# Moving one product of the normalisation to GpSimd, earlier weight pieces, and part of the first constant products in array halves

## The chip, the cores and the metric

One core of one Trainium2 chip runs the whole program: five engines (TensorE, VectorE, ScalarE, GpSimd, and SyncE that issues transfers), each with its own instruction stream, and semaphores between them. The metric is the time of one execution on the device in microseconds; the comparison uses the median of several runs.

## What is computed

The reference is a chain of three parts over 2304 tokens of width 512, all in float32.

```python
# 1: linear attention, 4 batches, 8 heads, 576 tokens, head size 64, 128 features
proj = x @ w_phi ; proj -= max(abs(proj)) ; phi = [exp(proj), exp(-proj)]
out = phi(q) @ (phi(k).T @ v) / (phi(q) @ sum(phi(k)) + 1e-6)
# 2: one of 8 experts per token (argmax of x @ w_gate)
x = gate * sigmoid(...) * (relu(x @ w1[e]) @ w2[e])          # 512 -> 1024 -> 512
# 3: RMS norm and a gated FFN
xn = x / sqrt(mean(x * x) + 1e-6) * rms_g                    # rms_g: one factor per feature
y  = (silu(xn @ w_gate) * (xn @ w_val)) @ w_out              # 512 -> 1536 -> 512
```

With these inputs only three experts are chosen by any token.

## The kernel before

Every large product is made of three products of split operands: a value is stored as a high part (rounded, type fp32r) and a low part (value minus high part), and high*high, high*low and low*high are added in PSUM. ScalarE writes high parts, VectorE writes low parts. So each tile that TensorE reads has passed ScalarE and then VectorE.

**Start.** `keep_warm(n)` (line 774) issues n products of a constant tile `warm` with 512 columns each; their results are never read. Twelve stand before the first slot of attention, eight between slots 0 and 1, eight between slots 1 and 2 (lines 779 to 786). The first slot waits for loads, for the split of `w_phi` and for the first tile of k.

**Attention** runs in slots, one per 128 tokens of k or q; rows are scattered to DRAM by expert in the end.

**Experts.** Tokens of an expert are taken in tiles of 288 (G). One tile is one *step*; there are eight steps g = 0 to 7 in this run, step 0 ahead of the routing table, then three *turns* (one per expert) of one, four and two steps. In a step TensorE goes through eight chunks m of 128 hidden rows: `hidden(m)` (12 products, lines 833 to 835), then `outputs(m-2)` (12 products, lines 846 to 848). `hidden(m)` needs VectorE's `relu_low(m-2)`, `outputs(m)` needs `relu_low(m)`. The next tile is transposed in four parts: `next_transpose` 0 and 1 after `hidden(7)`, 2 and 3 after `outputs(5)`; part 2 goes to the PSUM bank of part 0 and so waits until `take_rows` has read part 0 on ScalarE and VectorE. `once` (a turn's start) waits until all eight weight pieces of the turn are split.

**Weight pieces.** The next expert's weights are split in eight pieces during the first step of a turn (`split_step`, with `split` given): ScalarE `split_high` (line 975), VectorE `split_low` (line 1317), one piece at each of chunks 0 to 5 and two behind the last `take_rows`. Two such steps are in the experts' stage: g = 1 and g = 2. GpSimd issues the loads: `raw_in(2, ...)` (line 613) for the second matrix of the turn after the next once all eight pieces are split.

**Normalisation of tile n = g-1** runs inside step g in the same streams:
- ScalarE `copy_out` (1051): PSUM to `x2g` [128, 4, 288], at the start of the step.
- GpSimd `add_squares` (581, 584, 587): squares and two sums; TensorE `sum_squares` (854) after `hidden(4)`; VectorE `mean` (1386) at chunk 3; ScalarE `root` (1056) at chunk 3.
- VectorE `normal` at chunk 4: `reciprocal` (1391), then four products x2g * g * inverse root in place (1397).
- ScalarE `normal_high` at chunk 5: one copy of 1152 elements to `xoH` (1062). VectorE `normal_low` at chunk 5: `xoL` = x2g - xoH (1405).
- SyncE `rows_out` (465, 468, 472): stores xoH, then xoL, then the token numbers (a DRAM to DRAM transfer of 4 byte elements).

**Entry to the FFN.** The FFN's weights are twelve blocks of [128, 3, 512]. Blocks 0 and 1 pass through the buffer `stage[0]`, block 2 through `stage[1]`, which lies where expert weights were. SyncE's order after the loop is written by hand:

```python
e.wait_ge(s["pe_s1"], last * FC + 1)
block_in(0)                       # stage[0]
e.wait_ge(s["xst"], total * 32)
group_in(0)                       # first 384 tokens
e.wait_ge(s["pl_b"], 2)           # block 0 split, stage[0] free
block_in(1)
rows_out(prior)                   # tile 6
e.wait_ge(s["pe_s2"], total * FC + 2)
e.dma_start(stage[1], ffn_w[2])
for i in range(3, NF): block_in(i)    # each waits for bk_lo >= i - 2
```

GpSimd splits block 0 (lines 644, 646) behind its last step; ScalarE and VectorE split the others (1137, 1549) between the parts of group 0. `ffn_up(i)` (926 to 928, 24 products) waits for block i, `ffn_down(i-1)` (940 to 942) follows it. Six groups of 384 tokens, twelve blocks each, fill the rest of the time.

Of the kernel before, what the change touches and what calls it, by code (L numbers as in the profile page):

```python
# [25 lines left out]
P = 128  # L26
# [15 lines left out]
G = 288  # L42
# [16 lines left out]
def build_program(nc, q, k, v, w_phi, wg, wog, w1, w2, ffn_w, rms_g, out):  # L59
# [8 lines left out]
    with ctx:  # L68
# [88 lines left out]
        def sb(name, shape, dt=F32):  # L157
# [80 lines left out]
            "normalised, split, stored; token numbers stored, read": "dve_xn act_xh dve_xl xst idst id_in id_c",  # L238
# [84 lines left out]
        split_slots_dve = [(B - 1, sl) for sl in (1, 2, 3, 6, 8, 9)] + [(B, 0), (B, 1)]  # L323

# [50 lines left out]
        def _(e):  # L375
# [82 lines left out]
            def rows_out(n):  # L458
# [7 lines left out]
                e.wait_ge(s["dve_xl"], n + 2)  # L466
# [58 lines left out]
        def _(e):  # L525
# [93 lines left out]
            def step(par, g):  # L619
                add_squares(g - 1)  # L620
                gate_rows(g + 1)

            def split_step(pair, par, g):
# [3 lines left out]
                gate_rows(g + 1)  # L627
                with e.If(has_turn(pair * 2 + (par + 2))):
# [6 lines left out]
            with e.If(early > 0):  # L635
                e.sem_inc(s["pl_sq"], 1)
                e.sem_inc(s["pl_s0"], 1)
                e.sem_inc(s["pl_ss"], 1)
            with e.If(early < 1):
                gate_rows(0)  # L640
# [7 lines left out]
            add_squares(total_steps(e) - 1)  # L648
# [8 lines left out]
        def _(e):  # L657
# [120 lines left out]

            e.wait_ge(s["c_warm"], 1)
            keep_warm(12, (YM, YM + 1, YM + 2, YM + 3))  # L780
# [3 lines left out]
            keep_warm(8)  # L784
# [181 lines left out]
        def _(e):  # L966
# [101 lines left out]
            def step(par, g, split=None):  # L1068
                table(ACT.Sqrt)
                copy_out(g - 1)  # L1070
                for m in range(FC):
                    if m == FC - 1:
                        take_rows(g + 1, XT_BANK, (0, 1))
                    relu(g, m)
                    if split is not None and m < FC - 2:
                        split(m)
                    if m == 3:
                        root(g - 1)
                    if m == 5:
                        normal_high(g - 1)  # L1080
# [51 lines left out]
            def block_high(i):  # L1132
                if i == NF - 1:
                    e.wait_ge(s["dve_xl"], total + 1)
# [50 lines left out]
        def _(e):  # L1185
# [202 lines left out]
            def normal(n):  # L1388
# [3 lines left out]
                e.wait_ge(s["pl_sq"], n + 2)  # L1392
                settle(e, "carry_dve")
                e.wait_ge(s["dve_R"], n + 2)
                settle(e, "carry_dve")
# [3 lines left out]
                last.then_inc(s["dve_xn"], 1)  # L1399

            def normal_low(n):
# [6 lines left out]
            e.sem_inc(s["dve_r"], 2)  # L1408
            over_batches(e, slot, NJ)
# [6 lines left out]
            with e.If(early > 0):  # L1416
                take_rows(0, XT_FIRST)
                for name in ("dve_ms", "dve_R", "dve_xn", "dve_xl"):
# [90 lines left out]
            def step(par, g, split=None):  # L1509
                for m in range(FC):  # L1510
                    if m == FC - 1:
                        take_rows(g + 1, XT_BANK, (0, 1))
                    relu_low(g, m)
                    if split is not None and m < FC - 2:
                        split(m)
                    if m == 3:
                        mean(g - 1)
                    if m == 4:
                        normal(g - 1)
                    if m == 5:  # L1520
                        normal_low(g - 1)
# [99 lines left out]
```

## Time and profile before

| what | value |
|---|---|
| median of 3 runs | 951.33 us (948.44, 951.33, 953.78) |
| the profiled execution's own time | 948.03 us |
| span of its instructions | 946.4 us |
| TensorE busy | 927.0 us, 98% |
| VectorE, ScalarE, GpSimd busy | 440.6, 303.6, 118.5 us |
| stages by TensorE's lines | attention to 259 us, experts 259 to 486, FFN 487 to 940 |

The span counts from the first to the last instruction; 1.6 us of the execution lie around it. Busy times of the other engines say little here, since each of them works in short bursts that TensorE may or may not wait for. What is read are TensorE's waits, and for each of them what the other engines and the transfer queue did just before.

### The profile page before, as it was taken

The numbers are of one execution on the slowest core, as the hardware profiler recorded it, in microseconds if no ns is written. First come the engines' busy times: TensorE is split into PE (matmuls) and PEld (weight loads), VectorE is DVE, ScalarE is ACT, GpSimd is POOL, SyncE is SP. The second block draws the span as 40 slices with busy tenths as digits, with TensorE's granted clock in tenths as the row PEclk, the third lists the DMA queues.
The fourth block names the chain that finished last, engine by engine and source line by source line (L and its number), as shares of the span: only waits on it lengthen the run. The fifth ranks groups of instructions, "written<-read, shape, count | busy, mean of one in ns | idle before, by whom it ended". The sixth has DMA issues, their size and how long they took to land.

```text
span 946.4 us, 16281 instructions
## 1 busy us (share of the span) xinstructions
PE 927.0 (98%) x6240; PEld 888.4 (94%) x6241; DVE 440.6 (47%) x869; ACT 303.6 (32%) x491; POOL 118.5 (13%) x135
## 2 busy tenths in 40 slices
PE   8999999999999899999999999999999999999996
PEld 7999999999999899999999899999999999999995
DVE  5667767678565764433356642222222222222221
ACT  4444444465315553222344422112112112112111
POOL 1000210201333311222420001001001001001001
PEclk9999999999999999999999999999999999999999
DMA  9620821500154843333753360011002002000000
GB/s 266 183 59 1 299 80 54 146 1 34 46 182 137 190 84 72 70 39 61 175 150 134 133 185 34 1 34 67 1 1 100 0 0 100 0 0 34 1 1 33
DMA packets 52960, 75.35 MB, mean 80 GB/s; under 512 B 26512, under 2 KB 42512, under 8 KB 51248
## 3 DMA queue, kind: packets, MB, share of 16 engines
q1 hardware_dynamic: 46816, 56.07, 23.3%
q0 software_dynamic: 3488, 17.85, 5.2%
q10 hardware_dynamic: 2608, 0.79, 0.4%
q8 instruction: 31, 0.51, 0.2%
q14 instruction: 17, 0.14, 0.0%
HBM read 51.06 MB, written 23.64 MB: 79 GB/s over the span
## 4 chain that ended last, share of the span: by engine, by line
PE 91%; DVE 3%; DMA 2%; ACT 2%; issue 2%; POOL 0%; POOLq 0%; SPq 0%; DVEq 0%; ACTq 0%
PE ps L926 10%; PE ps L928 10%; PE ps L927 10%; PE ps L696 8%; PE ps L713 7%; PE ps L941 5%; PE ps L942 5%; PE ps L940 5%; PE ps L833 3%; PE ps L834 3%; PE ps L846 3%; PE ps L835 3%; PE ps L848 3%; PE ps L847 3%; PE ps L670 3%; PE ps L672 2%
## 5 line engine op out<-in xcount | busy, mean ns | idle before, releaser
L926 PE MATMUL ps<-xnH,blkH 128*128 128x384 f32 x576 | 193.8, 337 | 1.4 <-issue 1.0
L928 PE MATMUL ps<-xnH,blkL 128*128 128x384 f32 x576 | 193.6, 336 | 0.0
L927 PE MATMUL ps<-xnL,blkH 128*128 128x384 f32 x576 | 193.4, 336 | 0.0
L1556 DVE TENSOR_TENSOR sg<-sg,ps 128x384 f32<-128x384 f32 x72 | 39.9, 554 | 247.5 <-ACT sg L1142 247.5
L1142 ACT ACTIVATE sg<-ps 128x384 f32<-128x384 f32 x72 | 35.4, 491 | 254.2 <-PE ps L928 254.2
L926 PEld LDWEIGHTS ps<-xnH,blkH 128*128 128x128 f32 x576 | 108.3, 188 | 5.6 <-issue 2.7
L927 PEld LDWEIGHTS ps<-xnL,blkH 128*128 128x128 f32 x576 | 108.3, 188 | 2.7
L928 PEld LDWEIGHTS ps<-xnH,blkL 128*128 128x128 f32 x576 | 108.3, 188 | 0.0
L940 PE MATMUL ps<-blkH,hH 128*128 128x512 f32 x216 | 84.6, 392 | 0.9 <-DVE hL L1560 0.9
L941 PE MATMUL ps<-blkL,hH 128*128 128x512 f32 x216 | 84.9, 393 | 0.0
L942 PE MATMUL ps<-blkH,hL 128*128 128x512 f32 x216 | 84.9, 393 | 0.0
L833 PE MATMUL ps<-xmH,w1H 128*128 128x288 f32 x256 | 77.3, 302 | 5.9 <-DVE hmL L1379 3.3
L846 PE MATMUL ps<-hmH,w2H 128*128 128x288 f32 x256 | 78.7, 307 | 0.0
L834 PE MATMUL ps<-xmL,w1H 128*128 128x288 f32 x256 | 76.8, 300 | 0.0
L835 PE MATMUL ps<-xmH,w1L 128*128 128x288 f32 x256 | 76.6, 299 | 0.0
L848 PE MATMUL ps<-hmH,w2L 128*128 128x288 f32 x256 | 75.7, 296 | 0.0
L847 PE MATMUL ps<-hmL,w2H 128*128 128x288 f32 x256 | 75.7, 296 | 0.0
L1192 DVE TENSOR_REDUCE mx<-ps 128x4 f32<-128x512 f32 (+1 forms) x80 | 54.8, 685 | 42.6 <-PE ps L672 42.3
L713 PE MATMUL ps<-kvs,ex 128*128 128x65 f32 (+1 forms) x640 | 71.8, 266 | 0.5 <-DVE x L1233 0.5
L652 POOL DMA_INDIRECT out_dram<-ysb,idI x18 | 17.4, 969 | 430.7 <-ACT ysb L1157 427.4
L713 PEld LDWEIGHTS ps<-kvs,ex 128*128 128x128 f32 (+1 forms) x640 | 69.2, 184 | 1.3 <-issue 1.2
L1379 DVE SCALAR_TENSOR_TENSOR hmL<-ps,hmH 128x288 fp32r<-128x288 f32 x64 | 29.2, 456 | 84.7 <-ACT hmH L1046 84.2
(197 smaller groups left out, 1658.8 us busy)
## 6 DMA issues: line engine op xcount, KB each, us to landing
stage<-in_ffn_w SPq DMA_DIRECT2D x12, 768.0 KB, 4.6
xin<-xs_dram SPq DMA_DIRECT2D x9, 578.2 KB, 10.1
xs_dram<-zrow SPq DMA_DIRECT2D x8, 578.2 KB, 8.1
qT<-in_q SPq DMA_DIRECT2D x4, 1152.0 KB, 6.5
xnH_dram<-xoH SPq DMA_DIRECT2D x8, 576.0 KB, 3.4
xnL_dram<-xoL SPq DMA_DIRECT2D x8, 576.0 KB, 5.3
xnH<-xnH_dram SPq DMA_DIRECT2D x6, 768.0 KB, 5.2
xnL<-xnL_dram SPq DMA_DIRECT2D x6, 768.0 KB, 6.3
```

Source lines behind the costliest of these rows:

```text
L713: last = e.matmul(NUM[0:n, h // 4, h % 4, :], ex[:, at[1] % 2, sign, h, 0:n], kvs[:, 2 * h + sign, :], start=(sign == 0), stop=(sign == 1))
L833: e.matmul(o, w1H[par][:, c, cols], xmH[:, c, :], start=(c == 0), stop=False)
L834: e.matmul(o, w1H[par][:, c, cols], xmL[:, c, :], start=False, stop=False)
L835: last = e.matmul(o, w1L[par][:, c, cols], xmH[:, c, :], start=False, stop=(c == KC - 1))
L846: e.matmul(o, w2H[par][:, m, cols], hmH[:, m % 2, :], start=(m == 0), stop=False)
L847: e.matmul(o, w2H[par][:, m, cols], hmL[:, m % 2, :], start=False, stop=False)
L926: e.matmul(o, hi, xnH[par][:, c, :], start=(c == 0), stop=False)
L927: e.matmul(o, hi, xnL[par][:, c, :], start=False, stop=False)
L928: last = e.matmul(o, lo, xnH[par][:, c, :], start=False, stop=(c == KC - 1))
L940: e.matmul(o, hH[:, i % 2, tok], blkH[i][:, 2, :], start=(i == 0), stop=False)
L941: e.matmul(o, hH[:, i % 2, tok], blkL[i][:, 2, :], start=False, stop=False)
L942: last = e.matmul(o, hL[:, i % 2, tok], blkH[i][:, 2, :], start=False, stop=(i == NF - 1))
```

## The change

- The four products of `normal` become one product on GpSimd (`normalise`), x2g * inverse root, in place, after `gate_rows` in GpSimd's step. VectorE keeps the reciprocal (`inverse`), now at chunk 5.
- The factor g moves into the last split: `normal_high` is four ScalarE instructions with a scale, `normal_low` four VectorE instructions (x2g * g) - xoH; both stand at the end of the step, behind `take_rows(2, 3)`. So `copy_out` of the next step waits for `normal_low` (`dve_xl`).
- The eight pieces stand at chunks 1 to 6 (`PIECES_AT`); none is left behind the last `take_rows`. `root` moves to chunk 4.
- Start: `keep_warm(12)` becomes `keep_warm(8)` and `keep_warm_tiles(3)`; the first `keep_warm(8)` between slots becomes `keep_warm(3)` and `keep_warm_tiles(3)`.
- In the FFN's group 0 VectorE does `inverse` where it did `normal`; GpSimd does `normalise` of the last tile behind its `add_squares`.

```diff
+        PIECES_AT = {1: (0,), 2: (1, 2), 3: (3,), 4: (4, 5), 5: (6,), 6: (7,)}
@@ SyncE, rows_out
-                e.wait_ge(s["dve_xl"], n + 2)
+                e.wait_ge(s["dve_xl"], n + 3)
@@ GpSimd
+            def normalise(n):
+                e.wait_ge(s["dve_R"], n + 2)
+                settle(e, "carry_pool")
+                e.tensor_tensor(x2g[:, :, :], x2g[:, :, :], rinv[:, :].unsqueeze(1).to_broadcast([P, KC, G]), ALU.mult)\
+                    .then_inc(s["pl_xn"], 1)
             def step(par, g):
                 add_squares(g - 1)
                 gate_rows(g + 1)
+                normalise(g - 1)
             def split_step(pair, par, g):
                 add_squares(g - 1)
                 with e.If(has_turn(pair * 2 + (par + 2))):
                     raw_in(1, pair * 2 + (par + 2), pair * (2 * PIECES) + ((par + 1) * PIECES + KC))
                 gate_rows(g + 1)
+                normalise(g - 1)
                 with e.If(has_turn(pair * 2 + (par + 2))):
                     raw_in(2, pair * 2 + (par + 2), pair * (2 * PIECES) + (par + 2) * PIECES)
...
-            add_squares(total_steps(e) - 1)
+            total = total_steps(e)
+            add_squares(total - 1)
+            normalise(total - 1)
@@ TensorE
+            def keep_warm_tiles(n):
+                plain = warm[:, :].bitcast(F32)
+                for _ in range(n):
+                    for at in (0, D):
+                        e.matmul(ps[at:at + D, XL, 0:P], plain[:, 0:D], plain[:, 0:P], start=True, stop=True)
+                for _ in range(n):
+                    for at in (0, D):
+                        e.matmul(ps[:, XL - at // D, 0:2 * P], warm[at:at + D, 0:P], warm[at:at + D, 0:2 * P],
+                                 start=True, stop=True)
-            keep_warm(12, (YM, YM + 1, YM + 2, YM + 3))
+            keep_warm(8, (YM + 3, XL))
+            keep_warm_tiles(3)
...
             slot(0, 0)
-            keep_warm(8)
+            keep_warm(3)
+            keep_warm_tiles(3)
             slot(0, 1)
@@ ScalarE
             def copy_out(n):
                 e.wait_ge(s["pe_s2"], n * FC + (FC + 2))
+                e.wait_ge(s["dve_xl"], n + 2)
...
-                e.wait_ge(s["dve_xn"], n + 2)
+                e.wait_ge(s["pl_xn"], n + 2)
                 e.wait_ge(s["xst"], n * 32 + 64)
-                e.activation(xoH[:, :, :], x2g[:, :, :], ACT.Copy).then_inc(s["act_xh"], 1)
+                for c in range(KC):
+                    last = e.activation(xoH[:, c, :], x2g[:, c, :], ACT.Copy, scale=gcol[:, c:c + 1])
+                last.then_inc(s["act_xh"], 1)
...
                 for m in range(FC):
+                    relu(g, m)
+                    if m == 4:
+                        root(g - 1)
+                    if split is not None:
+                        for n in PIECES_AT.get(m, ()):
+                            split(n)
+                    if m == FC - 2:
                         take_rows(g + 1, XT_BANK, (0, 1))
...
                 take_rows(g + 1, XT_BANK, (2, 3))
-                if split is not None:
-                    split(FC - 2)
-                    split(FC - 1)
+                normal_high(g - 1)
@@ VectorE
-                for c in range(KC):
-                    last = e.scalar_tensor_tensor(out=x2g[:, c, :], in0=x2g[:, c, :], scalar=gcol[:, c:c + 1],
-                                                  in1=rinv[:, :], op0=ALU.mult, op1=ALU.mult)
...
-                e.tensor_tensor(xoL[:, :, :], x2g[:, :, :], xoH[:, :, :].bitcast(F32), ALU.subtract)\
-                    .then_inc(s["dve_xl"], 1)
+                for c in range(KC):
+                    last = e.scalar_tensor_tensor(out=xoL[:, c, :], in0=x2g[:, c, :], scalar=gcol[:, c:c + 1],
+                                                  in1=xoH[:, c, :].bitcast(F32), op0=ALU.mult, op1=ALU.subtract)
+                last.then_inc(s["dve_xl"], 1)
...
                 for m in range(FC):
                     relu_low(g, m)
+                    if m == 5:
+                        inverse(g - 1)
+                    if split is not None:
+                        for n in PIECES_AT.get(m, ()):
+                            split(n)
                     if m == 3:
                         mean(g - 1)
+                    if m == FC - 2:
+                        take_rows(g + 1, XT_BANK, (0, 1))
                 take_rows(g + 1, XT_BANK, (2, 3))
+                normal_low(g - 1)
```

## Rows read from the trace of the kernel before

**Rows 1.** Waits of TensorE, whole span: who waits for whom, us in total, times, longest
```profile
PE ps L833 <- DVE hmL L1379: 3.3, 2, 2.0
...
PE ps L833 <- DVE w2L L1317: 1.2, 1, 1.2
...
PE ps L926 <- DVE blkL L1549: 0.3, 1, 0.3
```

**Rows 2.** Timeline of GpSimd, last expert step: start us, us, instruction, [idle before]
```profile
460.26 2.11 POOL L581 TENSOR_TENSOR sq<-x2g 128x1152 f32<-128x1152 f32 x1 [20.08 <-ACT x2g L1051]
462.55 1.43 POOL L584 TENSOR_TENSOR sq<-sq 128x576 f32<-128x576 f32 x1 [0.18 <-POOL sq L581]
...
469.54 1.47 POOL L644 CAST blkH<-stage 128x1536 fp32r<-128x1536 f32 x1
471.10 3.50 POOL L646 TENSOR_TENSOR blkL<-stage,blkH 128x1536 fp32r<-128x1536 f32 x1
```

**Rows 3.** Timeline of VectorE, last expert step
```profile
473.17 1.95 DVE L1391 RECIPROCAL rinv<-rinv 128x288 f32<-128x288 f32 x1
475.27 1.81 DVE L1397 SCALAR_TENSOR_TENSOR x2g<-x2g,gcol,rinv 128x288 f32<-128x288 f32 x4 [0.16 <-DVE rinv L1391]
476.99 0.45 DVE L1379 SCALAR_TENSOR_TENSOR hmL<-ps,hmH 128x288 fp32r<-128x288 f32 x1
```

**Rows 4.** Timeline of ScalarE, last expert step: relu of chunk 5
```profile
475.56 0.41 ACT L1046 ACTIVATE hmH<-ps 128x288 fp32r<-128x288 f32 x1 [2.79 <-PE ps L848]
```

**Rows 5.** Timeline of TensorE: first product of the FFN, first of block 2
```profile
487.15 0.41 PE L926 MATMUL ps<-xnH,blkH 128*128 128x384 f32 x1 [1.02 <-issue]
...
497.70 0.41 PE L926 MATMUL ps<-xnH,blkH 128*128 128x384 f32 x1
```

**Rows 6.** Timeline of SyncE's transfers, entry to the FFN: start us, us of issue
```profile
478.77 0.62 SPq L465 DMA_DIRECT2D xnH_dram<-xoH  x1
...
481.03 0.63 SPq L472 DMA_DIRECT2D ids_dram<-xs_dram  x1
486.23 0.34 SPq L507 DMA_DIRECT2D stage<-in_ffn_w  x1
```

**Rows 7.** Block 1, token numbers, block 2: KB, us from issue to landing
```profile
stage<-in_ffn_w SPq DMA_DIRECT2D x1, 768.0 KB, 4.3
...
ids_dram<-xs_dram SPq DMA_DIRECT2D x1, 1.1 KB, 9.1
...
stage<-in_ffn_w SPq DMA_DIRECT2D x1, 768.0 KB, 8.0
```

**Rows 8.** Timelines of ScalarE and VectorE: block 2's high part, block 1's low part
```profile
494.27 1.49 ACT L1137 ACTIVATE blkH<-stage 128x1536 fp32r<-128x1536 f32 x1 [0.46 <-DMA stage<-in_ffn_w]
...
488.12 1.76 DVE L1549 TENSOR_TENSOR blkL<-stage,blkH 128x1536 fp32r<-128x1536 f32 x1 [3.99 <-ACT blkH L1137]
```

**Rows 9.** Timelines of GpSimd and VectorE, step g = 1
```profile
303.94 2.03 POOL L574 TENSOR_SCALAR xin<-xin 96x512 f32<-96x512 f32 x3
...
304.41 2.64 DVE L1317 TENSOR_TENSOR w2L<-w2raw,w2H 128x1024 fp32r<-128x1024 f32 x1 [0.49 <-ACT w2H L975]
...
311.17 1.21 DVE L1317 TENSOR_TENSOR w2L<-w2raw,w2H 128x1024 fp32r<-128x1024 f32 x1
```

**Rows 10.** Timeline of TensorE: g = 1: transposes 0 and 1, transposes 2 and 3; start of the last turn
```profile
313.01 0.66 PE L798 MATMUL ps<-ident,xin 96*128 96x96 f32 x6
...
315.13 0.58 PE L798 MATMUL ps<-ident,xin 96*128 96x96 f32 x5
...
431.48 0.40 PE L833 MATMUL ps<-xmH,w1H 128*128 128x288 f32 x1 [0.47 <-issue]
```

**Rows 11.** Timeline of TensorE, start: constant products; then the second slot's second half
```profile
9.48 2.01 PE L777 MATMUL ps<-warm 128*128 128x512 f32 x8
...
12.39 0.38 PE L670 MATMUL ps<-wbdH,tH 128*128 128x256 f32 x1 [0.19 <-DVE pm L1199]
```

**Rows 12.** A window in attention: us, busy times PE, PEld, DVE, ACT, POOL (instructions), clock, DMA
```profile
187.60:191.00 3.40, 3.40 (x19) 3.40 (x17) 1.38 (x2) 1.18 (x2) 0.00 (x0) 0.50 0.02 5
```

More of the change, by code:

```diff
@@ L237, in build_program @@
                 "act_x2 pl_sq pl_s0 pl_ss pe_SS dve_ms act_rt dve_R",
-            "normalised, split, stored; token numbers stored, read": "dve_xn act_xh dve_xl xst idst id_in id_c",
+            "normalised, split, stored; token numbers stored, read": "pl_xn act_xh dve_xl xst idst id_in id_c",
             "FFN weights: loaded (one per staging buffer), split (the first block's on its own)":
@@ L638, in _ @@
                 e.sem_inc(s["pl_ss"], 1)
+                e.sem_inc(s["pl_xn"], 1)
             with e.If(early < 1):
@@ L1071, in step @@
                 for m in range(FC):
-                    if m == FC - 1:
-                        take_rows(g + 1, XT_BANK, (0, 1))
[L1074 to L1080, printed above, removed]
+                    relu(g, m)
[5 more added lines that the diff above has]
+                    if m == FC - 2:
+                        take_rows(g + 1, XT_BANK, (0, 1))
                 take_rows(g + 1, XT_BANK, (2, 3))
-                if split is not None:
-                    split(FC - 2)
-                    split(FC - 1)
+                normal_high(g - 1)
             def split_step(pair, par, g):
@@ L1133, in block_high @@
                 if i == NF - 1:
-                    e.wait_ge(s["dve_xl"], total + 1)
+                    e.wait_ge(s["dve_xl"], total + 2)
                     settle(e, "carry_act")
@@ L1386, in mean, with inverse @@
                 e.tensor_scalar(rinv[:, :], ps[:, RB, 0:G], 1.0 / DM, 1e-6, ALU.mult, ALU.add).then_inc(s["dve_ms"], 1)
-            def normal(n):
+            def inverse(n):
                 e.wait_ge(s["act_rt"], n + 2)
                 e.reciprocal(rinv[:, :], rinv[:, :]).then_inc(s["dve_R"], 1)
[L1392 to L1395, printed above, removed]
-                for c in range(KC):
-                    last = e.scalar_tensor_tensor(out=x2g[:, c, :], in0=x2g[:, c, :], scalar=gcol[:, c:c + 1],
-                                                  in1=rinv[:, :], op0=ALU.mult, op1=ALU.mult)
-                last.then_inc(s["dve_xn"], 1)
             def normal_low(n):
@@ L1417, in _ @@
                 take_rows(0, XT_FIRST)
-                for name in ("dve_ms", "dve_R", "dve_xn", "dve_xl"):
+                for name in ("dve_ms", "dve_R", "dve_xl"):
                     e.sem_inc(s[name], 1)
@@ L1510, in step @@
                 for m in range(FC):
-                    if m == FC - 1:
-                        take_rows(g + 1, XT_BANK, (0, 1))
                     relu_low(g, m)
-                    if split is not None and m < FC - 2:
-                        split(m)
+                    if m == 5:
[3 more added lines that the diff above has]
+                            split(n)
                     if m == 3:
                         mean(g - 1)
[L1518 to L1521, printed above, removed]
+                    if m == FC - 2:
+                        take_rows(g + 1, XT_BANK, (0, 1))
                 take_rows(g + 1, XT_BANK, (2, 3))
-                if split is not None:
-                    split(FC - 2)
-                    split(FC - 1)
+                normal_low(g - 1)
             def split_step(pair, par, g):
@@ L1571, in group @@
                         if i == 3:
-                            normal(total - 1)
+                            inverse(total - 1)
                         if i == 5:
```

1 line of the change is left out of this document (added).

## The prediction, made before the changed kernel was run

> **What bounds the kernel now.** I read four views, in this order. The page's busy times first: TensorE has 927.0 of 946.4 us, so only what delays TensorE counts, and little can be won. The waits of TensorE second [rows 1]: in the experts' stage it waits twice, 3.3 us in all (the longer 2.0, so the other 1.3), for VectorE's low part of the hidden rows, in the two steps that also split weights, and once, 1.2 us, for the last weight piece; in the FFN 0.3 us for a block. That is 4.8 us, the most that the change's aim can give. Third, the timelines at the entry to the FFN [rows 2 to 8], since the change puts new work on GpSimd there and SyncE's hand-written order waits for GpSimd. Fourth, the step with weight pieces [rows 9, 10] and the start [rows 11].
>
> **Entry to the FFN, the largest term.** The FFN's block 0 is split by GpSimd behind its last step. Before, its work there is done early: the high part at 469.54, the low part from 471.10 to 474.60 [rows 2]. With the change `normalise` of tile 6 stands ahead of it, and that waits for the reciprocal of the last step.
> - When the reciprocal ends: ScalarE's relu of chunk 5 runs 475.56 to 475.97 [rows 4], VectorE's low part takes 0.45, so 476.4, then 1.95 [rows 3]: 478.4. It was at 475.1, since it stood at chunk 4.
> - What `normalise` costs on GpSimd: no row shows it. The subtraction with two inputs took 3.50 for 1536 elements, the sum of two halves 1.43 for 576 [rows 2]; a line through both gives 1.43 + 576/960 * 2.07 = 2.67 for 1152. Lower bound 2.11, the square of the same 1152 elements from one input [rows 2]; upper bound 3.6, twice VectorE's 1.81 for the same product [rows 3]. I take 2.67, between its two nearest rows of two inputs. It ends at 481.1.
> - Block 0 then: 1.47 + 3.50 and 0.1 between [rows 2], so 486.2 in place of 474.60, 11.6 later. TensorE begins the FFN at 487.15 after 1.02 us in which it waited for nothing that the profile shows [rows 5]: covered, with 0.9 to spare.
> - Block 1 is the first loss. Its load waits for block 0 to leave the buffer: issue 486.2, landing 4.3 later [rows 7] at 490.5, high part 1.49, low part 1.76 [rows 8], ready at 493.8 (before 489.9). TensorE wants it after block 0's 24 products: between the two rows of [rows 5] it did 48 products of 384 columns and 9 of 512, 23040 columns in 10.55 us, so 24 of 384 take 4.2 and block 1 is wanted at 491.3. Stall 2.5.
> - Block 2 is the second. SyncE issues it behind `rows_out(6)`, and that now stands behind the wait of block 1's load. xoH goes out some 1.2 later at 487.4 (an estimate: about half the 2.26 between the issues of xoH and the token numbers), the numbers 2.26 after it at 489.7 [rows 6]. Before, the numbers landed 9.1 after their issue, at 490.1, and block 2, in the queue behind them since 486.23, at 494.2, that is 4.1 behind them [rows 6, 7]; ScalarE waited for it [rows 8]. Now: numbers landed at 498.8, block 2 at 502.9, split at 506.2. Before it was split at 497.5 (494.27 + 1.49 + 1.76) and TensorE took it at 497.70 without a gap. So 506.3 in place of 497.70: **+8.6**, the 2.5 of block 1 within it.
> - Bounds: 2.5 if block 2 doesn't wait behind the numbers (issue 490.5, landing 494.8, split 498.1, which the 2.5 already covers); 9.5 with the 3.6 for `normalise`.
> The Trainium skill, "GPSIMD Engine Reference", section Engine selection, sends elementwise products of two inputs to VectorE and has GpSimd at about half its speed; by that the product is the 3.6 of the upper bound and the sum 0.9 more. This case's rows put the price lower, no run has shown it yet.
>
> **The two steps with weight pieces.** VectorE loses the four products (1.81) from the chunks where it is late, and `normal_low` goes to the step's end. It gains pieces 6 and 7 there, 1.21 each [rows 9], for which it was free behind the last `take_rows` before. Let R be the end of the low part of chunk 5, on which `hidden(7)` waits. In its stream follow reciprocal 1.95, piece 6 1.21, low part of chunk 6 0.45, piece 7 1.21, low part of the first rows, of one chunk's size, 0.45: R + 5.3. GpSimd's work beside it is not free: beside `gate_rows` a piece took 2.64 in place of 1.21 [rows 9], so 1.4 more, and `normalise` now runs exactly beside pieces 6 and 7: R + 6.7. TensorE needs that low part for transposes 2 and 3: `hidden(7)` first, 1.6 (twelve products; twelve with six transposes take 2.12), then 2.12 from the first transposes to the second [rows 10]: R + 3.7. So the wait moves: not at `hidden(7)` any more but at transpose 2, up to 3.0, less what R comes ahead of the moment when TensorE wants it, which adding up chunks 4 and 5 puts at 0.3 to 0.5. I take 2.5 in each of two steps, 5.0 in place of 3.3: +1.7. The turn's start gains: pieces are all split, what is left is the overhead that the last turn's start shows (0.47 idle of its own [rows 10]) in place of 1.2: -0.7. Sum **+1.0**. Bounds: -4.0 (no wait left but that overhead) and +3.0 (another 1.4 from `gate_rows`, which slides to chunk 4 as SyncE's `rows_out` now waits for `normal_low` ahead of `rows_next`, and 0.6 in step 2).
> GpSimd issues the load of the second matrix (`raw_in(2)`) earlier, as all pieces are split before the step's end, though behind `normalise`; step 2 gets it in time. The other steps: `normal_high` (four times 0.41, overlapped) and `normal_low` (four times 0.45) lie behind `take_rows` and run under `outputs(6)`, `outputs(7)` and the first products of the next step; `copy_out` then ends about when ScalarE can begin relu 0. Cost nothing; if that cover goes, up to 0.3 in each of five steps. SyncE sends for the rows of the next tile later, since it waits for `normal_low` first; they are still gated ahead of `normalise`, and so ahead of the transposes.
>
> **FFN, group 0.** VectorE is 1.81 shorter ahead of block 6, whose low part TensorE waited 0.3 for [rows 1]: **-0.3**, bounds -0.7 and 0.
>
> **Start.** The first set is over before k's first tile is split, and TensorE idles there; the longer list fills that idle time: 0, at most +1.0 at the low clock. Second set: eight products of 512 columns took 2.01 with the last one's way through the pipe, 1.7 of issue, 0.21 each [rows 11]. Now three (0.64), six float32 ones of 128 columns and six of 256. In series, at float32's four passes, that is 6 * 0.21 + 6 * 0.11 = 1.9, in all 2.6: 0.85 more. 0.39 of it vanishes in the gap before the second half [rows 11] (0.19 idle and the rest of a start): **+0.5**. Bounds -0.1 and +1.2 (0.3 for each change of form unseen in the trace).
> The Trainium skill, "TensorEngine Tiling (Array Packing)", section Key Properties, says that tiles of the array run load and product in parallel; by that the second set takes 1.6 and this term is -0.1. No product of the trace before uses two halves at once, so the rows can't weigh it; TensorE's records will.
>
> **Sum** against the profiled execution's own 948.03: 8.6 + 1.0 - 0.3 + 0.5 = +9.8, 957.8. That execution lies 3.3 below the median of the three runs, 951.33. Part of the spread is the clock: three stretches of 3.41 us in attention and at the experts' start ran at 0.50 of full clock, 1.2 GHz in place of 2.4 [rows 12], each 1 to 1.7 us lost, and which stretches fall so need not repeat. The forecast is for the median: **961.1**. A measurement of this kernel can tell about 0.5% (4.8 us) from no change: below 946.6 and above 956.1.
>
> **Rivals.**
> - A, the forecast: blocks 1 and 2 both late. 0.65, 957 to 965.
> - B: the token numbers do not hold back block 2. For: they are 1.1 KB, and another pattern of the queue could let block 2 pass. Against: block 2 landed 8.0 after issue, 3.7 more than block 1 [rows 7]. Then 2.5 + 1.0 - 0.3 + 0.5 = +3.7, 955.0. 0.14.
> - C, the other side, not slower: GpSimd's product doesn't slow VectorE and the low part of the first rows comes by R + 3.7. The place is transpose 2 of steps 1 and 2, the price -4.0 in place of +1.0, and it decides the sign once the FFN's entry costs less than 4.3, so with B: 2.5 - 4.0 - 0.3 + 0.0 = -1.8, 949.5; if block 1 is early too, 947. For: VectorE is relieved of 1.81 where it was late. Against: 5.3 is over 3.7 even with no collision. 0.09.
> - D: the half-array products don't hold the clock, and the first slots run at 1.2 GHz for one more stretch of 3.41 us: +1.7 on A, or +3 with the shifted stretches of attention. For: the clock fell where TensorE's products were short [rows 12]. 0.12, 963 to 965.
>
> **Numbers.** Predicted 961.0. Range 953 to 966: from B less a microsecond or two to D. Faster by over 0.5%: 0.05 (C's better end and luck with the clock); within: 0.18 (B and the rest of C); slower: 0.77 (A, D, little of B).
>
> **What would show it.** Right: GpSimd's new product near 2.7 us at about 19.6 into a step; block 1 issued at about 27.5 into the last step in place of 15.9; TensorE waiting for `blkL` twice, some 2.5 and 6; ScalarE waiting for the `stage` transfer; a wait on the first rows' low part ahead of line 798 in steps 1 and 2; no w2L wait. Wrong: one wait of 2.5 only (B), none (block 0 still early), or no wait at line 798.

## The result, and the profile after

| kernel | median us | lowest to highest | runs |
|---|---|---|---|
| before | 952.34 | 948.44 to 953.78 | 4 |
| changed | 963.85 | 963.17 to 964.23 | 4 |

The row of before has the three runs given above and one more. The ratio is 1.0127, 95% interval 1.0094 to 1.0159: slower, by 11.5 us at the medians. The forecast was 961.0 in a range of 953 to 966. The profiled execution took 964.23. The changed kernel was timed once more later, beside others (below, changed_again): 959.17, ratio 1.0098.

The page of the changed kernel: span, busy times, and the slices with the granted clock.

```profile
span 962.5 us, 16361 instructions
...
PE 936.6 (97%) x6267; PEld 897.4 (93%) x6268; DVE 433.4 (45%) x861; ACT 307.9 (32%) x515; POOL 140.5 (15%) x143
...
PEclk9999999999799999999998999999999999999999
```

TensorE is busy for 936.6 of 962.5 us: 9.6 us more busy and 6.5 us more idle than before. The products are the same but for the start, so nearly all of the 9.6 is time at the lower clock, and the waits of TensorE (to be read against [rows 1]) hold the rest.

```profile
PE ps L953 <- DVE blkL L1568: 7.1, 2, 4.6
PE ps L825 <- DVE xmL L1400: 4.4, 2, 2.5
...
PE ps L860 <- issue: 1.4, 2, 1.0
PE ps L953 <- POOL blkL L658: 1.0, 1, 1.0
```

The waits of `hidden` for the hidden rows' low part (3.3) and for the weight piece (1.2) are gone, and so is the 0.3 at block 6. Two waits for the blocks of the FFN (7.1) and two for the low part of the next tile's first rows (4.4) stand in their place. The entry to the FFN, in the timelines of GpSimd, SyncE and ScalarE (against [rows 2, 6, 8]), and block 1 and 2 on TensorE (against [rows 5]):

```profile
484.53 2.66 POOL L595 TENSOR_TENSOR x2g<-x2g,rinv 128x1152 f32<-128x1152 f32 x1 [2.14 <-DVE rinv L1418]
487.13 1.47 POOL L656 CAST blkH<-stage 128x1536 fp32r<-128x1536 f32 x1
488.68 3.51 POOL L658 TENSOR_TENSOR blkL<-stage,blkH 128x1536 fp32r<-128x1536 f32 x1
```
```profile
492.22 0.36 SPq L489 DMA_DIRECT2D stage<-in_ffn_w  x1
494.42 0.62 SPq L467 DMA_DIRECT2D xnH_dram<-xoH  x1
...
496.31 0.66 SPq L474 DMA_DIRECT2D ids_dram<-xs_dram  x1
497.18 1.17 SPq L509 DMA_DIRECT2D stage<-in_ffn_w  x1
```
```profile
496.55 1.49 ACT L1164 ACTIVATE blkH<-stage 128x1536 fp32r<-128x1536 f32 x1 [3.62 <-DMA stage<-in_ffn_w]
...
509.28 1.48 ACT L1164 ACTIVATE blkH<-stage 128x1536 fp32r<-128x1536 f32 x1 [7.85 <-DMA stage<-in_ffn_w]
```
```profile
493.18 0.41 PE L953 MATMUL ps<-xnH,blkH 128*128 128x384 f32 x1 [1.01 <-POOL blkL L658]
500.18 0.66 PE L953 MATMUL ps<-xnH,blkH 128*128 128x384 f32 x1 [2.58 <-DVE blkL L1568]
```

The product on GpSimd takes 2.66 and pushes the split of block 0 to 487.13 to 492.2. TensorE takes it at 493.18, after 1.01 of idle time where it had 1.02 before [rows 5], so that itself costs nothing. Block 1's load leaves at 492.22, when that buffer is free, and TensorE takes block 1 at 500.18, after 2.58 of waiting. The token numbers leave at 496.31, block 2's load right behind them at 497.18, and ScalarE has it at 509.28. From issue to landing (against [rows 7]):

```profile
ids_dram<-xs_dram SPq DMA_DIRECT2D x1, 1.1 KB, 10.5
stage<-in_ffn_w SPq DMA_DIRECT2D x1, 768.0 KB, 12.1
```

TensorE reaches block 2 at 512.70 after 4.55 of waiting. From the FFN's first product to block 2 it took 19.52 us; before, 10.55 [rows 5].

**Where the 16.1 us of span went**, by TensorE's marks (the start of the experts, of the FFN, of block 2, the last product): up to the experts +3.5 (262.98 against 259.46), experts +2.5 (230.20 against 227.69), entry to block 2 +9.0, the rest +1.1. The windows at half clock account for most of the parts outside the entry; the last two lie within it or reach out of it.

```profile
185.90:189.30 3.40, 3.40 (x19) 3.40 (x17) 1.38 (x2) 0.78 (x2) 0.00 (x0) 0.50 0.00 0
247.30:257.50 10.20, 10.20 (x62) 9.71 (x61) 2.42 (x5) 1.19 (x2) 3.09 (x4) 0.50 0.00 0
261.00:267.80 6.80, 6.80 (x36) 6.54 (x35) 4.62 (x21) 1.86 (x5) 0.81 (x2) 0.50 0.37 89
349.70:353.10 3.40, 3.40 (x18) 3.32 (x17) 1.51 (x4) 2.92 (x7) 0.00 (x0) 0.51 0.00 0
499.90:503.30 3.40, 3.12 (x10) 3.15 (x11) 1.68 (x3) 0.52 (x1) 3.22 (x2) 0.50 1.42 136
510.20:517.00 6.80, 4.30 (x14) 4.33 (x15) 4.77 (x5) 2.83 (x4) 0.00 (x0) 0.50 0.37 136
```

The column behind the five engines is the granted clock as a share of 2.4 GHz. So 34 us of the span ran at 1.2 GHz, in the profile before 10.2 ([rows 12] is one of its three stretches). Three of these stretches began while TensorE waited or just after (349.70, 499.90, 510.20); the others lie where the change touches nothing.

### The profile page after: what moved, and what is told of

Read it like the earlier page. It is cut to its first block, busy times and chain, and to the rows that moved or that the text cites. A ratio compares the mean times of both kernels' runs of the same rounds, so it can differ in the third digit from the quotient of the medians.

```text
span 962.5 us, 16361 instructions
## 1 busy us (share of the span) xinstructions
PE 936.6 (97%) x6267; PEld 897.4 (93%) x6268; DVE 433.4 (45%) x861; ACT 307.9 (32%) x515; POOL 140.5 (15%) x143
## 4 chain that ended last, share of the span: by engine, by line
PE 92%; issue 2%; DMA 2%; DVE 2%; ACT 1%; POOL 1%; SPq 0%; POOLq 0%; DVEq 0%; ACTq 0%
PE ps L953 10%; PE ps L955 10%; PE ps L954 10%; PE ps L710 7%; PE ps L727 7%; PE ps L968 5%; PE ps L969 5%; PE ps L967 5%; PE ps L860 3%; PE ps L862 3%; PE ps L861 3%; PE ps L873 3%; PE ps L875 3%; PE ps L874 3%; PE ps L684 3%
## 5 line engine op out<-in xcount | busy, mean ns | idle before, releaser
L953 PEld LDWEIGHTS ps<-xnH,blkH 128*128 128x128 f32 x576 | 109.4, 190 | 12.4 <-issue 9.5
L727 PE MATMUL ps<-kvs,ex 128*128 128x65 f32 (+1 forms) x640 | 74.3, 272 | 0.0
L727 PEld LDWEIGHTS ps<-kvs,ex 128*128 128x128 f32 (+1 forms) x640 | 71.5, 190 | 0.9 <-issue 0.8
```

The source lines that it names most:

```text
L727: last = e.matmul(NUM[0:n, h // 4, h % 4, :], ex[:, at[1] % 2, sign, h, 0:n], kvs[:, 2 * h + sign, :], start=(sign == 0), stop=(sign == 1))
L953: e.matmul(o, hi, xnH[par][:, c, :], start=(c == 0), stop=False)
```

## The experiments

All ratios are against the kernel before, timed beside each of them in four sessions (medians 948.59, 950.94, 950.45 and 953.89; 17 to 29 runs each). "At equal clock" is explained under changed_again: it takes the run-to-run clock out, its unit is us above the kernel before, and its 95% intervals reach 0.4 to 0.8 to either side (0.2 for new_start_alone). The last column is from one profile of each kernel. quarter_product leaves work out, so its result is not that of the others.

| kernel | median us, runs | ratio (95%) | at equal clock | TensorE's waits for blocks; for first rows or hidden rows |
|---|---|---|---|---|
| changed_again | 959.17, 12 | 1.0098 (1.0067 to 1.0128) | +6.7 | 6.2; 4.2 |
| late_block0 | 958.46, 6 | 1.0096 (1.0067 to 1.0124) | +6.6 | 6.4; 2.7 |
| block2_ahead | 953.74, 10 | 1.0051 (1.0021 to 1.008) | +3.1 | 2.6; 4.1 |
| block0_first | 962.26, 7 | 1.0103 (1.0062 to 1.0144) | +5.4 | 6.1; 4.3 |
| rows_first | 956.47, 10 | 1.0058 (1.0028 to 1.0089) | +3.8 | 6.4; 0.4 |
| quarter_product | 955.28, 4 | 1.0068 (1.0041 to 1.0095) | +2.5 | 6.1; 0.7 |
| pieces_alone | 951.38, 10 | 1.0012 (0.998 to 1.0044) | +2.6 | 0.3; 5.8 |
| old_start | 960.99, 4 | 1.0116 (1.0066 to 1.0167) | +6.3 | 5.4; 4.0 |
| new_start_alone | 948.77, 10 | 0.9993 (0.9963 to 1.0023) | +0.2 | 0.3; 2.7 |
| all_three | 949.72, 10 | 0.9991 (0.9955 to 1.0026) | +0.6 | 3.4; 0.3 |
| tile6_behind_3 | 947.97, 12 | 0.9971 (0.9942 to 0.9999) | 0.0 | 3.1; 0.6 |
| tile6_behind_5 | 948.94, 12 | 0.9952 (0.9925 to 0.998) | -3.3 | none; 0.3 |

### Entry to the FFN

**late_block0**: the kernel before, with nothing of the change but the lateness of block 0.

```diff
+            late = total_steps(e)
+            e.wait_ge(s["dve_xl"], late)
+            settle(e, "carry_pool")
             e.wait_ge(s["st_0"], 16)
             e.tensor_copy(blkH[0][:, :, :], stage[0][:, :, :]).then_inc(s["pl_b"], 1)
```

> Kernel before, with one edit: GpSimd waits for the low part of tile 6 before it splits the FFN's block 0, so the split starts near 479.9 and ends near 485 in place of 474.6, still ahead of the moment when TensorE wants it. If the queue behind block 0 is the cause (block 1's load behind the split, block 2's load behind the token numbers), TensorE waits about 1.5 to 2.5 us for block 1 and 3.5 to 5 for block 2, and the kernel takes 5 to 8 us more than the kernel before, with no part of the change in it. If the late product itself or something else of the change makes the loss, it stays within 1 us of the kernel before.

Measured: 1.0096, and 6.6 at equal clock beside the 6.7 of the changed kernel. Block 0's split begins at 481.94 in place of 469.54 [rows 2]. The waits and the load of block 2:

```profile
PE ps L929 <- DVE blkL L1552: 6.4, 3, 4.7
PE ps L836 <- DVE hmL L1382: 2.7, 2, 2.0
```
```profile
502.66 1.48 ACT L1140 ACTIVATE blkH<-stage 128x1536 fp32r<-128x1536 f32 x1 [6.50 <-DMA stage<-in_ffn_w]
```

TensorE waits 1.4 at block 1 and 4.7 at block 2, with the product still on VectorE. So it is the time at which block 0 leaves its buffer that costs, through the chain of transfers behind it, whatever makes it late.

**block2_ahead**: the changed kernel, with block 2's load issued ahead of the stores of tile 6.

```diff
             block_in(1)
-            rows_out(prior)
             e.wait_ge(s["pe_s2"], total * FC + 2)
             settle(e, "carry_sp")
             e.dma_start(stage[1][:, :, :], ffn_w[2]).then_inc(s["st_1"], 16)
+            rows_out(prior)
```

> Changed kernel, with block 2's load issued right behind block 1's, ahead of the stores of tile 6 and its token numbers. If block 2 is late only because it queues behind the token numbers, its load lands some 5 us after its issue near 492.6, ScalarE no longer waits for it, and TensorE keeps only block 1's wait of about 2.6: 4.5 us less than the changed kernel from the wait and 1 to 3 more from the low clock that follows it. If block 2 were late for another reason (ScalarE or VectorE busy, the transfer itself slow), at most 1 us is won.

Measured: the second wait is gone, the first stays.

```profile
PE ps L825 <- DVE xmL L1400: 4.1, 2, 2.5
PE ps L953 <- DVE blkL L1568: 2.6, 1, 2.6
```

The entry took 14.89 (488.63 to 503.52) in place of 19.52, and the time fell by 3.6 at equal clock. The stores of tile 6 hold back the load behind them; rival B, by which block 2 would pass, falls.

This run moves all three stores, xoH and xoL of 576 KB each with the 1.1 KB of token numbers, and no run moves the numbers alone. In the changed kernel xoL itself took 10.6 from issue to landing (505.9), so the runs do not tell the three apart. The trace before tells more. There xoL had landed at 484.8 (issued at 480.02, 4.8 to landing), 1.4 before block 2's load was issued, and only the numbers were on their way, to 490.1; the load still took 8.0 where block 1's took 4.3 [rows 6, 7]. From 487.9 to 492.1 the 16 DMA engines were busy 45% of the time and moved 53 GB/s, from 492.1 to 494.5 they moved 405. So the bulk of the stores is not the cause there. The numbers are the likely one, but that was not shown by leaving them out.

**block0_first**: the changed kernel, with block 0's split inside the last step, after `gate_rows` and ahead of `normalise`, under a condition on the step's number.

```diff
             def step(par, g):
                 add_squares(g - 1)
                 gate_rows(g + 1)
+                block_0(g)          # split of block 0, if g is the last step
                 normalise(g - 1)
```

> Changed kernel, with block 0's split ahead of the new product in the last step alone. If GpSimd's order is the root of the entry's loss, block 0 is split by about 487.5 (5 after the rows are gated at 482.4), block 1 goes out some 4.5 us before TensorE's last expert product, and TensorE waits 0 to 1 us for block 1; block 2 still queues behind the token numbers, whose issue now follows the product that has moved back by about 2.5 (xoH near 493), so its wait stays at 4 to 7. So 2 to 4 us are won over the changed kernel, not all 7 to 9. If the order is not the root, nothing is won.

Measured: the wait at block 1 is gone (500.65 after 496.40, 4.25 as before), the one at block 2 grew from 4.6 to 6.1, and the entry took 16.77. Block 1 in time alone brings 1.3 at equal clock, with 0.8 to either side, less than the 2 to 4 expected: what TensorE no longer waits at block 1 it waits at block 2, which hangs on the stores of tile 6, and these on `normalise`. The two blocks are one chain, as the forecast put it ("the 2.5 of block 1 within it").

### The two steps with weight pieces

The steps of the changed kernel, on VectorE, GpSimd and TensorE in step g = 1 (against [rows 9, 10]):

```profile
314.50 1.16 DVE L1344 TENSOR_TENSOR w2L<-w2raw,w2H 128x1024 fp32r<-128x1024 f32 x1
315.58 0.44 DVE L1406 SCALAR_TENSOR_TENSOR hmL<-ps,hmH 128x288 fp32r<-128x288 f32 x1
315.94 3.29 DVE L1344 TENSOR_TENSOR w2L<-w2raw,w2H 128x1024 fp32r<-128x1024 f32 x1
319.15 0.81 DVE L1400 TENSOR_TENSOR xmL<-ps,xmH 128x288 fp32r<-128x288 f32 x2
```
```profile
314.76 3.39 POOL L595 TENSOR_TENSOR x2g<-x2g,rinv 128x1152 f32<-128x1152 f32 x1 [4.62 <-DVE rinv L1418]
```
```profile
319.74 0.80 PE L825 MATMUL ps<-ident,xin 96*128 96x96 f32 x6 [2.53 <-DVE xmL L1400]
```

Piece 7 takes 3.29 beside the product on GpSimd, where piece 6 just ahead took 1.16, and the product 3.39 in place of 2.66. The first rows' low part stands behind piece 7, and TensorE's transposes 2 and 3 wait 2.53 for it.

The records show in which way. Piece 6 ran beside the product too, from its start at 314.76 to 315.66, and was no longer for it. Piece 7 begins at 315.94, in the middle of the product; the product ends at 318.15 and piece 7 at 319.23, 1.08 later, which is nearly its whole length. Step g = 2 shows the same, 347.86 and 348.94 (start and duration of each added up):

```profile
344.45 3.41 POOL L595 TENSOR_TENSOR x2g<-x2g,rinv 128x1152 f32<-128x1152 f32 x1 [1.93 <-DVE rinv L1418]
345.63 3.31 DVE L1344 TENSOR_TENSOR w2L<-w2raw,w2H 128x1024 fp32r<-128x1024 f32 x1
```

So does the piece beside `gate_rows` before, 305.97 and 307.05 [rows 9]. By these records the two take turns: what begins second gets on at about the time when the other ends, and its price is what was then left of the other. No run was made for this alone. The short low part between the pieces (315.58), which reads PSUM, kept its 0.44.

**rows_first**: the changed kernel, with `take_rows(0, 1)` ahead of piece 7, on ScalarE and VectorE alike.

```diff
+                    if m == FC - 2:
+                        take_rows(g + 1, XT_BANK, (0, 1))
                     if split is not None:
                         for n in PIECES_AT.get(m, ()):
                             split(n)
-                    if m == FC - 2:
-                        take_rows(g + 1, XT_BANK, (0, 1))
```

> Changed kernel, with the first two parts of the next rows taken ahead of piece 7. If the wait at the transposes (2.5 and 1.9 us) comes from VectorE's queue, it goes, perhaps 0.5 us comes back at the second last output chunk, and the time falls by 3 to 4.5 us against the changed kernel. If it comes from the rows' load or from GpSimd's gating, it stays.

Measured: both waits of 2.5 and 1.9 are gone, 0.35 at `outputs(6)` and 0.82 at the turn's start are left, and 2.8 us are saved at equal clock. The entry's waits stay at 6.4.

**quarter_product**: the changed kernel, with the product on one of the four chunks of `x2g` (`x2g[:, 0:1, :]`, 288 elements in place of 1152); the other three leave the normalisation without the inverse root.

> Changed kernel with GpSimd's product on one of four chunks of the tile; the other three chunks leave without the inverse root. The product falls from 2.66 to about 0.8 us. If it slows the weight pieces beside it, piece 7 (3.3 us on VectorE) falls to 1.2 to 1.9 and the wait at the transposes from 2.5 and 1.9 to about 0.5 to 1 each. Block 0 is split 1.9 earlier, so block 1's wait falls from 2.6 to about 0.8; block 2's follows by up to 1.9. In all 4 to 6 us less than the changed kernel. If GpSimd and VectorE don't disturb each other, the wait at the transposes changes by under 0.5.

Measured, in step g = 1:

```profile
308.16 1.56 POOL L595 TENSOR_TENSOR x2g<-x2g,rinv 128x288 f32<-128x288 f32 x1 [4.62 <-DVE rinv L1418]
```
```profile
309.34 1.46 DVE L1344 TENSOR_TENSOR w2L<-w2raw,w2H 128x1024 fp32r<-128x1024 f32 x1
```

With 1.6 us of product in place of 3.4, piece 7 took 1.46 (it ended at 310.80, again 1.08 behind the product) and TensorE waited 0.7 once in place of 4.4: the length of the product beside the pieces makes the wait, not the new order of VectorE's work by itself. At the entry block 1's wait fell to 1.8, and block 2's stayed at 4.4, since the stores are still behind block 1's load; the expectation had it fall as well.

**pieces_alone**: the kernel before, with `PIECES_AT` as in the change and nothing else; the four products stay on VectorE.

> Kernel before with only the weight pieces at chunks 1 to 6; the product, the copies and the start as before. VectorE then has pieces 4 and 5, the reciprocal, the four products and piece 6 between two low parts. If moving pieces needs the product moved too, the wait at hidden 7 grows from 2.0 and 1.3 to 3.5 to 5 each, and the wait of 1.2 for the last piece goes: 3 to 6 us slower than the kernel before. If the pieces' place is what gains, it is 1 us faster or level.

Measured: 1.0012, within the noise, and 2.6 at equal clock, short of the 3 to 6 expected. There is no wait for the weight piece any more, but 5.4 in four waits at `hidden` in place of 3.3 in two, and 0.4 at the transposes.

```profile
PE ps L835 <- DVE hmL L1379: 5.4, 4, 3.1
```

The earlier pieces need room on VectorE in the very chunks where it is late. The product's move makes that room, and the collision fills it again.

### The start

**new_start_alone** (the kernel before with the new lists of constant products) and **old_start** (the changed kernel with the old ones):

```diff
-            keep_warm(12, (YM, YM + 1, YM + 2, YM + 3))
+            keep_warm(8, (YM + 3, XL))
+            keep_warm_tiles(3)
...
-            keep_warm(8)
+            keep_warm(3)
+            keep_warm_tiles(3)
```

> Kernel before with only the new constant products. Same two theories from the other side: within 0.5 us of the kernel before if only their length counts; 3 to 5 us slower, with more stretches at the low clock in attention, if they shift or weaken what keeps the clock up.

> Changed kernel with the constant products of the kernel before (12 and 8 of full width). The half-array products ran in pairs 6 ns apart and the later slots start within 0.2 us of before, so if only their length counts the time stays within 0.5 us of the changed kernel. If they are what puts more of attention's end at the low clock (17 us at 0.50 between 247 and 268 in the changed kernel, against 3.4 before), that goes and the time falls by 3 to 5 us.

Measured: 0.9993 alone, and 1.0116 without it. So far as these runs can tell, the start neither costs time nor lowers the clock: with the old lists the changed kernel still had 30.7 us at half clock in its profile. TensorE's records of the second set in the changed kernel (against [rows 11]):

```profile
9.62 0.85 PE L791 MATMUL ps<-warm 128*128 128x512 f32 x3
10.40 0.88 PE L798 MATMUL ps<-warm 128*64 128x128 f32 x12
11.21 0.63 PE L801 MATMUL ps<-warm 64*128 64x256 f32 x6
11.77 0.38 PE L684 MATMUL ps<-wbdH,tH 128*128 128x256 f32 x1
```

From 9.62 to 11.77 is 2.15, the third slot began at 15.15 in place of 15.04, and the first slot had already been 0.13 later (8.14 against 8.01).

### The clock

**changed_again**: the changed kernel once more, with more runs.

> The changed kernel itself, for more runs with their granted clock. If its loss is the waits plus a clock that falls more often, the slope of time over low clock time is near 0.42 as in the kernel before, the time at zero low clock is 6.5 to 7.5 us above that of the kernel before, and its mean low clock time is some 8 to 15 us above the other's 20. If the clock differs by chance alone, mean low clock times are alike and the ratio falls to 1.007.

Measured: 959.17 us median of 12 runs, from 953.9 to 965.8. The profiled execution of 953.86 has a granted clock of 0.993, that of the first measurement had 964.23 at 0.981, and both have the same waits (6.2 and 4.0 here, 7.1 and 4.4 there). Each run lists its mean granted clock, so the time at half clock can be worked out from it, about (1 - clock) * span * 2. Over the 89 runs of the kernel before in the four sessions, a run was longer by 0.41 us for each us at half clock, with 0.7 us of scatter left; for the 111 runs of the changed and the edited kernels the same fit gives 0.40. So 1 us at half clock costs 0.4, and 0.001 of mean clock 0.8 us of a run. "At equal clock" in the table takes this out: each kernel's mean time less 0.42 per us at half clock, against the same of the kernel before (0.42 is the fit over all 89 runs at once; 0.41 would change a row by less than 0.1).

By that the change costs 6.7 us. The figure is low, by an estimate of 1.5 us from this one profile: it takes 0.4 also for each us at half clock between the FFN's start and block 2 (3.7 us in this profile), where the loads set the end and not TensorE. The same holds for the other kernels that wait for blocks. What lies above that in a median is the clock outside. The kernel before had 19 to 22 us at half clock on average, the changed one 24.9 here, where 28 to 35 were expected, and 35.6 in its first four runs. The six others that keep block 2's wait or the late rows had 23 to 31, the rest 15 to 20, and among these is tile6_behind_3 with one wait of 3.1 and the lowest mean, 15.2. So long waits mostly go along with more time at half clock; it was not shown that they cause it. The stretches of this profile in and at the end of the entry, which took 18.70 (484.34 to 503.04):

```profile
492.40:495.80 3.40, 3.40 (x13) 3.40 (x12) 0.74 (x1) 0.23 (x1) 2.90 (x3) 0.50 0.70 49
502.70:506.10 3.40, 3.06 (x10) 3.09 (x11) 1.96 (x5) 1.90 (x2) 0.00 (x0) 0.50 0.62 213
```

### A version that keeps what the change was after

**all_three**: the changed kernel with block2_ahead, block0_first and rows_first together.

> Changed kernel with all three repairs: block 2's load ahead of tile 6's stores, block 0's split ahead of the product in the last step, the rows ahead of piece 7. If the waits named are all that the change adds, TensorE has none over 1 us left between 263 and 520 but the starts of turns, and the time is 3 to 5 us under the kernel before (944 to 946 beside 948.6). If something else was added, it stays level with the kernel before or above.

Measured: level with the kernel before, not 3 to 5 us below it. Blocks 1 and 2 are in time, but the stores of tile 6, now behind block 2's load, hold back blocks 3 and 4, for which TensorE waits 1.8 and 1.5.

**tile6_behind_3**: all_three with the stores of tile 6 behind block 3's load.

> As all_three, but the stores of tile 6 and its token numbers behind block 3's load. In all_three TensorE waited 1.8 us for block 3 and 1.5 for block 4. If both came from the queue behind the token numbers, they go (under 0.3 us each), and with the time at the low clock taken out (0.42 us per us, the slope over the runs so far) the kernel comes to 939 to 940 beside 942 of the kernel before: 2 to 3 us faster. If ScalarE and VectorE are what those blocks wait for, nothing changes against all_three (942.7).

Measured: the wait has moved to block 4. Its load left 2.2 behind the token numbers, and ScalarE waited for it:

```profile
PE ps L960 <- DVE blkL L1575: 3.1, 1, 3.1
```
```profile
505.85 1.48 ACT L1171 ACTIVATE blkH<-stage 128x1536 fp32r<-128x1536 f32 x1 [3.03 <-DMA stage<-in_ffn_w]
```

The 0.9971 was partly the clock: at equal clock it is level with the kernel before.

**tile6_behind_5**: the same, behind block 5's load.

```diff
             block_in(3)
+            block_in(4)
+            block_in(5)
             rows_out(prior)
-            for i in range(4, NF):
+            for i in range(6, NF):
                 block_in(i)
```

> The kernel tile6_behind_3, with SyncE storing tile 6 behind the issue of block 5's load in place of block 3's. In tile6_behind_3 block 4's load was issued at 492.57, 2.2 behind the token numbers, and ScalarE waited 3.03 for it; TensorE waited 3.1 (510 us). Theory (the token numbers hold back only the load right behind them, and the splits of blocks 4 and 5 are wanted sooner after their issue than that of block 6): block 5 is issued at about 498, the numbers at about 502, they land 10 later, block 6's load lands at 512 to 516 and is wanted by TensorE at 516 to 518, so TensorE waits for no block, or under 1 us once at block 6; TensorE's other waits stay. Time 3 us below tile6_behind_3: 0.990 to 0.997 of the kernel before, the runs' differing clock included. Rival (any load behind the numbers comes late, whichever block it is): 2 to 3 us of waiting stand at block 6, and the ratio is 0.995 to 1.000 as for tile6_behind_3.

Measured: 0.9952, 0.9925 to 0.998, faster than the kernel before clear of the noise. No wait for a block is left: what is left at the FFN is the 1.0 and the 0.9 that the kernel before has too, and one new wait of 0.5 for the rows of group 1, whose loads come behind.

```profile
PE ps L962 <- issue: 1.0, 1, 1.0
...
PE ps L962 <- DMA xnL<-xnL_dram: 0.5, 1, 0.5
```

The kernel before was itself slower here than in the other three sessions: 943.8 at equal clock, with more scatter, against 941.3 to 942.1. Taken by itself this kernel is 1.2 below tile6_behind_3 at equal clock (940.5 against 941.7), not 3.3. So the waits at the blocks are gone, but how much of the 3.3 would stand beside another session's kernel before is open.

ScalarE still waited 0.80 for block 6's load, which TensorE did not feel. By block 6 the loads run that far ahead of their use; at blocks 2 to 4 they do not.

## Why the prediction was right

The forecast was rival A, and its number and its mechanism held. Point by point:

- **Price of the product.** Taken 2.67 by the line through two rows, measured 2.66. The upper bound of 3.6 is the Trainium skill's half speed of VectorE, "GPSIMD Engine Reference", Engine selection, laid on VectorE's 1.81. That was the wrong row, since those are four instructions of another kind. Like against like the trace agrees with the page: a subtraction of 1536 elements took 3.50 on GpSimd and 1.76 on VectorE [rows 2, 8], and one of 1152 took VectorE 1.36 (line 1405), half of 2.66. In the split steps the product took 3.39 and 3.41, as it waited for VectorE's piece there.
- **Entry.** Forecast +8.6 to block 2, measured 19.52 less 10.55, +9.0. Counted from block 1's issue, block 2 was put at 20.1 (506.3 less 486.2) and came at 20.5 (512.70 less 492.22). Within it errors cancelled, which is luck: xoH was issued 2.2 behind block 1, not 1.2; the numbers took 10.5 to land, not 9.1; and block 2 was there no later than 2.5 behind them, not 4.1. Of the two waits 7.1 were seen where 8.6 stood, because TensorE, at half clock from 499.90 to 503.30, was itself later to ask for block 2: 19.52 less 7.1 is 12.4 for work that took 10.55 before. That 1.8 cost nothing more, since the loads set when block 2 was there. In changed_again the term is 18.70 less 10.55, +8.2.
- **Steps with pieces.** The wait moved where it was said, to transposes 2 and 3 of both steps, 2.5 and 1.9 against 2.5 each. R, the end of chunk 5's low part, was 312.71; the first rows' low part was done at R + 6.9 (R + 6.7 forecast), of which the collision made 2.1, not 1.4. The forecast carried the 1.4 over from `gate_rows`; what counted was how much of the product was left when piece 7 began (318.15 less 315.94). The turn's start had 0.1 of its own left in place of 0.5. So the waits sum to 4.5 after 4.5 before: the term is 0.0, where the forecast had +1.0, inside its bounds.
- **FFN, group 0.** The 0.3 at block 6 is gone, as said.
- **Start.** +0.1 where +0.5 was taken: mis-sized. The serial reckoning of the half-array products was wrong. Their records come in pairs that start 3 to 11 ns apart, one on each half. By the rule of the Trainium skill in "TensorEngine Tiling (Array Packing)", Key Properties, the set takes 1.6; here it took 2.15, and the 0.55 more is 0.15 to 0.2 for each of three changes of form. The rule was right as to the direction, and no row of before could have shown it.
- **The clock.** The sum put nothing on it but 3.3 from the profiled execution to the median. The measured terms sum to 9.0 + 0.0 - 0.3 + 0.1 = 8.8, near the forecast's 9.8 and the 8.7 between the medians of changed_again (959.17) and the kernel before beside it (950.45). The 11.5 of the first four runs is more, and their 35.6 us at half clock, 10.7 above changed_again's mean, are 4.3 us of it by the fit. That 961.0 lies close to both medians, 963.85 and 959.17, owes something to where the clock fell. Rival D had the right size for a wrong reason: the start does not lower the clock, as old_start shows.
- **C, the other side,** fell on the collision: with three quarters of the product gone, the wait for the low part shrank from 4.4 to 0.7.

## What to carry to other kernels

An engine that splits the first weight block early is the head of a chain: block 0's buffer, block 1's load, the stores behind it in the queue, block 2's load. Before giving such an engine new work ahead of that, follow the queue's order to the last load that TensorE needs soon, and put stores with a small scattered transfer among them where the load behind has a long way to its use. Before putting a GpSimd instruction beside VectorE's, look at which begins second, since that one may wait for what is left of the other. And before comparing two kernels by a few us, look at each run's clock: here it explains nearly all of the spread within a kernel, and taking it out shows differences of 1 to 3 us that the medians hide.

## What the runs showed that was not expected

- A store of token numbers of 1.1 KB took 9 to 11 us from issue to landing at the FFN's entry, and with the two stores of the tile ahead of it delayed the load issued 1 to 5 us behind it: block 2, then 3 and 4, then 4 alone, then 6, as the three were moved back. Only behind block 5 did no wait of TensorE come of it.
- Two engines held each other up by far more than the extra work: a VectorE piece of 1.2 took 3.29 beside a GpSimd product of 2.66, which took 3.39. In the four places named above the piece ended 1.08 behind GpSimd's last instruction, so it waited and did not merely run slower. `gate_rows` in step g = 2 took 4.04 where it took 2.84 in the same step before and 2.03 in step g = 1, as the pieces now run beside more of it.
- A quarter of the product took 0.80 in the steps without pieces, somewhat more than a quarter of 2.66, and 1.56 beside the pieces: by the same records the difference is waiting, not work.
- A us at half clock costs 0.4 us of the run, not the 0.5 of an engine that never waits. That part of such stretches lies where others set the end is the likely reason.
